# A gated linear attention feeding two feed-forward layers: removing the slot without scores and reordering the work of each slot

## What is computed

```python
mag = np.sqrt(a_re * a_re + a_im * a_im)
scale = np.minimum(mag, 0.999) / (mag + 1e-06)
for t in range(S):
    new_re = ar * S_re - ai * S_im
    new_im = ar * S_im + ai * S_re
    S_re, S_im = (new_re + kv, new_im)      # kv = outer(k_t, v_t)
    y[:, :, t] = einsum('bhd,bhde->bhe', q_t, S_re)
```

## Time and profile before

| what | us |
|---|---|
| median of 3 runs (lowest, highest) | 1066.19 (1065.41, 1066.72) |
| the profiled execution, its own time | 1071.88 |
| span of the profiled execution | 1070.2 |
| PE busy, share of the span | 91% |
| DVE, ACT, POOL busy | 60%, 47%, 29% |
| mean granted TensorE clock | 0.981 |

### The profile page before, as it was taken

How to read it: one execution, slowest core, us unless ns; L and a number is a source line. 1 busy time by engine, 2 the same in 40 slices (tenths; PEclk the granted TensorE clock), 3 DMA queues, 4 the chain that set the end, 5 groups by cost and what they waited for, 6 DMA issues and landing times.

```text
span 1070.2 us, 17927 instructions
## 1 busy us (share of the span) xinstructions
PE 970.4 (91%) x6882; PEld 949.3 (89%) x6882; DVE 646.3 (60%) x1116; ACT 500.5 (47%) x885; POOL 313.4 (29%) x291
## 2 busy tenths in 40 slices
PE   0377687999999999999999999999999999999998
PEld 0367686899999899998999999999999999999997
DVE  4856786888887888877887234553434434343432
ACT  5735665766666777666765354231212121212121
POOL 2213431222222222222222233333333333333332
PEclk9998798999999999998999999999999999999999
DMA  5470232334223333332222071010101010101000
GB/s 184 126 171 15 67 81 71 102 84 110 69 68 90 84 84 101 92 89 68 68 76 68 22 280 33 13 46 1 45 1 45 1 45 1 45 1 45 1 23 23
DMA packets 77862, 70.54 MB, mean 66 GB/s; under 512 B 32592, under 2 KB 73552, under 8 KB 77392
## 3 DMA queue, kind: packets, MB, share of 16 engines
q1 hardware_dynamic: 77456, 69.10, 23.0%
q10 hardware_dynamic: 320, 0.30, 0.2%
HBM read 40.90 MB, written 9.44 MB: 47 GB/s over the span
## 4 chain that ended last, share of the span: by engine, by line
PE 58%; DVE 16%; SPq 9%; ACT 8%; issue 5%; DMA 4%; DVEq 0%; ACTq 0%
PE op L1042 9%; PE op L1044 9%; PE op L1043 9%; PE hp L1042 9%; PE hp L1044 9%; PE hp L1043 9%; SPq L358 5%; SPq L361 4%; DMA st<-prod 3%; ACT gate L563 2%; DVE t_fb L742 2%; DVE gated L792 2%; DVE t_phase L714 2%; PE gp L1009 2%; DVE t_fb L730 2%
## 5 line engine op out<-in xcount | busy, mean ns | idle before, releaser
L463 POOL TENSOR_TENSOR g_lo<-gated,g_hi 128x384 fp32r<-128x384 f32 x256 | 277.1, 1082 | 669.0 <-ACT g_hi L570 669.0
L570 ACT ACTIVATE g_hi<-gated 128x384 fp32r<-128x384 f32 x256 | 134.4, 525 | 377.9 <-DVE gated L806 290.6
L802 DVE TENSOR_SCALAR gate<-hp,alpha_sb 128x384 f32<-128x384 f32 x128 | 79.1, 618 | 229.7 <-PE hp L1044 229.7
L792 DVE SCALAR_TENSOR_TENSOR gated<-gate,hp 128x384 f32<-128x384 f32 x128 | 70.6, 552 | 121.2 <-ACT gate L563 121.2
L1042 PE MATMUL hp<-x_hi,wa_hi 128*128 128x384 f32 x384 | 132.1, 344 | 10.1 <-DVE x_lo L770 7.4
L1042 PE MATMUL op<-g_hi,wb_hi 128*128 128x384 f32 x384 | 136.7, 356 | 1.8 <-ACT out_sb L575 1.1
L1044 PE MATMUL op<-g_hi,wb_lo 128*128 128x384 f32 x384 | 131.5, 343 | 0.0
L1043 PE MATMUL op<-g_lo,wb_hi 128*128 128x384 f32 x384 | 131.3, 342 | 0.0
L1042 PE MATMUL op<-g_hi,wa_hi 128*128 128x384 f32 x384 | 129.9, 338 | 0.7 <-issue 0.7
L1044 PE MATMUL hp<-x_hi,wa_lo 128*128 128x384 f32 x384 | 130.1, 339 | 0.0
L1043 PE MATMUL hp<-x_lo,wa_hi 128*128 128x384 f32 x384 | 129.9, 338 | 0.0
(11 more groups left out here) (98 smaller groups left out, 1851.8 us busy)
## 6 DMA issues: line engine op xcount, KB each, us to landing
st<-prod SPq DMA_DIRECT2D x94, 145.1 KB, 2.9
a_sb<-a_in SPq DMA_DIRECT2D x24, 288.0 KB, 3.8
qk_sb<-qk_in SPq DMA_DIRECT2D x24, 288.0 KB, 3.6
v_pad<-v_in SPq DMA_DIRECT2D x24, 192.0 KB, 3.6
x<-out_sb SPq DMA_DIRECT2D x8, 576.0 KB, 3.9
x_raw<-x SPq DMA_DIRECT2D x8, 576.0 KB, 4.5
out<-out_sb SPq DMA_DIRECT2D x8, 576.0 KB, 3.2
st<-prod SPq DMA_DIRECT2D x96, 32.2 KB, 1.9
```

The costliest lines, as they stand in the source:

```text
L463: pool.tensor_tensor(g_lo[:, at, :], gated[:, at * UT:(at + 1) * UT], g_hi[:, at, :].bitcast(F32), ALU.subtract).then_inc(glo_done, 1)
L570: act.activation(g_hi[:, at, :], gated[:, at * UT:(at + 1) * UT], ACT.Copy).then_inc(ghi_done, 1)
L792: dve.scalar_tensor_tensor(out=gated[:, to], in0=gate[:, at], scalar=1.0, in1=hp[:, n % 2, 0:UT], op0=ALU.min, op1=ALU.mult).then_inc(gate ...
L802: dve.tensor_scalar(gate[:, at], hp[:, n % 2, 0:UT], 0.0, alpha_sb[:, m:m + 1], ALU.min, ALU.mult).then_inc(gate_done, 1)
```

## The change

The slot without a chunk goes: chunk c has slot c, and there are slots -3 to 23. Slots 3, 4, 5 have 5, 5 and 6 items. On DVE, `phases` and `fractions` of the next chunk stand ahead of the slot's first `gate1`; in the early slots the five instructions of the chunk after next stand ahead of the masks. On ACT, `high` stands behind the attention's work of its position, and in the early slots `logs`, `inverses` and then both `copy_k` follow each other in position 1. On PE, an item that begins a unit issues its `hidden` before its `output`. The four DMAs of the second matrix are issued together behind `load_a(2)` in slot -2, and the splits are spread 3, 4, 4, 4, 5, 2, 2.

```diff
-W_LOADS = {-1: range(6, 8), 0: range(8, 10)}
-W_SPLITS = {-2: 3, -1: 3, 0: 3, 1: 3, 2: 4, 3: 4, 4: 4}
-ITEMS = {CPU: 4, CPU + 1: 4, CPU + 2: 3, CPU + 3: 5}
+W_SPLITS = {-2: 3, -1: 4, 0: 4, 1: 4, 2: 5, 3: 2, 4: 2}
...
 def chunk_at(s):
-    if s < CPU:
-        return s if s >= 0 else None
-    return s - 1 if CPU < s <= NCH else None
+    return s if 0 <= s < NCH else None
...
 def items_of(s):
...
+    u, j = divmod(s, CPU)
+    return list(range((u - 1) * MT_FF + MT_FF * j // CPU, (u - 1) * MT_FF + MT_FF * (j + 1) // CPU)) if u > 0 else []
...
@@ SP
-                    for w in W_LOADS.get(s, ()):
-                        load_w(w)
...
                     if c4 is not None and c4 >= 2:
                         load_a(c4)
+                    if c4 == 2:
+                        for w in range(6, 10):
+                            load_w(w)
...
@@ ACT
                 if n is not None:
                     gate_of(n + GSTEP)
-                if pos == 2 and c0 is not None and not early(s):
-                    x_high(c0)
-                if n is not None:
-                    high(n + GSTEP)
                 if pos == 0:
                     if keeps and not early(s):
                         copy_k(c0, 0)
                     if c1 is not None:
                         waves(c1)
-                    if keeps and early(s):
-                        copy_k(c0, 0)
                 if pos == 1:
-                    if keeps:
+                    if keeps and not early(s):
                         copy_k(c0, 1)
...
                     if c2 is not None:
                         logs(c2)
+                        if early(s):
+                            inverses(c2)
+                    if keeps and early(s):
+                        copy_k(c0, 0)
+                        copy_k(c0, 1)
                 if pos == 2:
-                    if c2 is not None:
+                    if c0 is not None:
+                        x_high(c0)
+                    if c2 is not None and not early(s):
                         inverses(c2)
-                    if c0 is not None and early(s):
-                        x_high(c0)
...
                 if pos == 4 and c2 is not None:
                     angle(c2)
+                if n is not None:
+                    high(n + GSTEP)
...
@@ DVE
+                if pos == 0 and c1 is not None:
+                    phases(c1)
+                    fractions(c1)
                 if n is not None:
                     gate1(n + GSTEP)
-                if pos == 0:
-                    if c1 is not None:
-                        phases(c1)
-                        fractions(c1)
-                    if c0 is not None and not early(s):
-                        mask(c0, 0)
-                        mask(c0, 1)
+                if pos == 0 and c0 is not None and not early(s):
+                    mask(c0, 0)
+                    mask(c0, 1)
...
-                    if c0 is not None and early(s):
-                        mask(c0, 0)
-                        mask(c0, 1)
-                if pos == (2 if early(s) else 3) and c2 is not None:
+                if pos == (1 if early(s) else 3) and c2 is not None:
                     residue(c2)
                     refine(c2)
                     ratio(c2)
-                if pos == (2 if early(s) else 4) and c2 is not None:
+                if pos == (1 if early(s) else 4) and c2 is not None:
                     lost(c2)
                     decays(c2)
+                if pos == 1 and c0 is not None and early(s):
+                    if c0 == 0:
+                        dve.wait_ge(masks_set, 4)
+                    mask(c0, 0)
+                    mask(c0, 1)
...
@@ PE
+            def first_half(n):
+                if n % MT_FF == 0 and n + HSTEP < 2 * N1:
+                    hidden(n + HSTEP)
+                else:
+                    output(n)
+
+            def second_half(n):
+                if n % MT_FF == 0:
+                    output(n)
+                elif n + HSTEP < 2 * N1:
+                    hidden(n + HSTEP)
...
                 if n is not None:
-                    output(n)
+                    first_half(n)
                 if pos == 0 and c0 is not None:
                     score(c0, 1)
                 if n is not None:
-                    hidden(n + HSTEP)
+                    second_half(n)
```

More of the change, by code:

```diff
@@ L69, in w2o_tiles @@
     return [k for k in ((2, 3) if m == 0 else (m + 3,)) if k < MT_FF]
-def slot_of(c):
-    return c if c < CPU else c + 1
 def chunk_at(s):
-    if s < CPU:
-        return s if s >= 0 else None
-    return s - 1 if CPU < s <= NCH else None
+    return s if 0 <= s < NCH else None
 def items_of(s):
[L84 to L90, removed]
+    u, j = divmod(s, CPU)
+    return list(range((u - 1) * MT_FF + MT_FF * j // CPU, (u - 1) * MT_FF + MT_FF * (j + 1) // CPU)) if u > 0 else []
 def splits_at(s, pos):
@@ L98, in places @@
 def places():
-    for s in range(FIRST_SLOT, NCH + 1):
+    for s in range(FIRST_SLOT, NCH):
         items = items_of(s)
@@ L833, in _ @@
             for s, pos, n, c0, c1, c2, c3 in places():
+                if pos == 0 and c1 is not None:
+                    phases(c1)
+                    fractions(c1)
                 if n is not None:
                     gate1(n + GSTEP)
-                if c0 == 0 and pos == 0:
-                    dve.wait_ge(masks_set, 4)
-                if pos == 0:
-                    if c1 is not None:
-                        phases(c1)
-                        fractions(c1)
-                    if c0 is not None and not early(s):
-                        mask(c0, 0)
-                        mask(c0, 1)
+                if pos == 0 and c0 is not None and not early(s):
+                    mask(c0, 0)
+                    mask(c0, 1)
                 if pos == 1:
@@ L1101, in _ @@
             for n in range(N1 - MT_FF, 2 * N1):
-                output(n)
-                if n + HSTEP < 2 * N1:
-                    hidden(n + HSTEP)
+                first_half(n)
+                second_half(n)
                 if n == N1 - MT_FF:
```

## The result

The changed kernel takes 1032.97 us (1032.25 to 1033.37) beside 1066.45 for the one before: ratio 0.9681, 95% interval 0.9660 to 0.9701. Its profiled execution took 1032.25 us, close to its median; that of the kernel before took 1071.88, 5.7 above its own first median.

A forecast was written before the change was run, and what follows sets the result against it. Early handovers between engines, then PE with waits for stack DMAs, were taken as the bound. 1071.88 - 10.7 - 9 - 5.7 = 1046.5 us, also 1066.19 - 19.7; range 1037 to 1062.

The forecast's parts named there:

- 10.7 us gained: Early slots, up to slot 6: its chunk would start at 181.0 instead of 191.70; bounds 14 and 3.
- 9 us: Later slots: shorter waits for stack DMAs, 8.7 from six waits behind units' first slots plus little in second slots.
- The five: Early slots, DVE's five instructions per chunk: taken at 3.8 us, with 2.8 and 4.6 as ends.
- the 46.0: Early slots: the time up to which nothing on DVE moves, the end of the factors of chunk 1.
- 68.5 reckoned: Slots 3 to 5, sixteen items and three chunks: 66.75 us plus 0.9 for a wait and 0.9 for four splits.
- 1.85 earlier: A unit's first slot: `forward` would come at 339.4, taking min(wait, 1.85) off each of six waits.
- 0.2 at most: A unit's second slot, where PE's hidden block sets the gate: gain for each of six, in us.
- The late high part: Rival, slower: `high` in a slot's second position comes too late and PE waits; 1088 at 2 us per slot, chance 0.07.
- slack of 2.2 us: A slot's second position: POOL's low part would end at 369.9, and PE wants it at 372.08.
- The prediction's 5.7: Two later slots behind waits, at clocks 0.93 and 0.87: 1.8 + 3.9 us over their like, expected to go.
- The lock rival: Early chain: three POOL splits block DVE's five or factors through the shared port, 3.8 us, giving 1050.3; chance 0.10.

The follow-up runs named there:

- x3: The changed kernel with ACT making the high part directly behind its gate again, ahead of the attention's work, in all positions: 1044.53 us.
- y2: The changed kernel with POOL filling the weights' low parts with zeros instead of subtracting two tiles, so those parts are missing from the result: 1027.83 us.

## Why the prediction was wrong in size

The sign and the shape of the chain were right, and two terms of the sum were too small by about the same. The early "10.7 us gained" was 17.4. The later "9 us" was 16.2 when the lowered clock is taken out (21.1 less 4.9). Together that is 13.9 us, and the median fell by 13.8 more than forecast.

- **Early slots.** The chain, its order and both of its idle stretches (ACT behind the stack DMAs, the first gate behind the angle) were right. The five were taken at 3.8 us; they took 2.7 (45.41 to 48.13) in each of three slots, since no split was running when one of them started: 3.3 us. The start was 0.6 earlier than the 46.0, the rest is in ACT's parts. The splits met the backward scan and `mags` instead. In sum chunk 3 came 4.6 us earlier than reckoned.
- **Slots 3 to 5.** 68.5 reckoned, 66.4 measured: of the two added terms (a wait of 0.9, splits 0.9) almost nothing showed. With the line above this is the 6.7 us that the early gain was short.
- **Later slots.** This is the step whose mechanism failed: "Together **9 us**". It gave the late high part no gain, only a cost ("ACT inserts `high` (0.5) ahead of the gate"), and so had `forward` 1.85 earlier. In the slot that it followed, `forward` came 3.1 earlier (8.10 to 4.99 behind the start), in the six first slots 2.1 to 3.7: with `high` undone, x3, `phases` starts 2.0 later and `forward` up to 2.0 later. And `end_floor` gave 0.63 in each of 20 chunks, which the prediction had not seen: the late `high` moves POOL's low part away from it. The six waits went, worth 9.1 as against 8.7; those behind second slots fell from 4.4 to 2.5, not by "0.2 at most" each; a wait of 0.7 at 333.14 went; and first slots got 3.0 us shorter apart from their waits, in part the waits for the eviction (0.25 and 0.84 us before), which the prediction left out although it named `leave`. The last 1.5 us are spread over other slots, at most 0.4 in each, and stay open.
- **The late high part** was the rival on the slow side. It is the opposite: x3 shows 11.6 us of gain hanging on it. Its slack of 2.2 us was reckoned well enough, PE never waited for POOL; what was missing is that the instructions it yields to are on the chain and POOL is not.
- **Clock.** Two slots at a lowered clock before, none between 6 and 23 after: 4.9 us of the 21.1 in the profile (24.55 and 26.64, less their waits, against 21.8). The prediction's 5.7 had left the waits in. Medians fell by 33.5 and the profiled executions by 39.6, so taking the 5.7 us off the median's gain was right by its size. That unprofiled runs lack just those drops is not shown: the mean clock was 0.981 in the profiled execution and 0.980 to 0.982 in runs of 1064.7 to 1070.0.
- **The lock rival** took place, 5 us by y2, but on other instructions than the ones named, and mostly as a cost that the kernel before has too (11.6 us of lengthened DVE instructions before, 10.6 after).

## What to carry to other kernels

When a slot's chain loops over several engines, subtract its length from the bound engine's work in each kind of slot: a delay costs nothing until the sum of delays passes that slack, so parts undone one by one can look nearly free: the high part moved back at single positions or pairs lost 4.4 us in sum, and at all positions 10.5. Put an instruction that has slack (here the high part) behind those on the chain, and look at what it starts on a third engine: here even a DVE instruction of 0.17 us lasted until POOL's subtraction ended, 0.6 us in every slot, and 0.8 beside a product where it was hidden. A slot with less work for the bound engine than the loop is long is not cheaper than a full one; merge it away.

## What was not expected of the hardware

An instruction on 128x3 elements, with one tile as its input, took 0.80 us instead of 0.17 beside a POOL subtraction of 1.13 to 1.15 us (75 times in four kernels), and a set of three scans 2.20 instead of 1.23 beside one of 1.26. A POOL fill of the same tile (0.53 us) beside the same scans changed nothing.
